# Attention and two mixtures of experts on one core: another place for the block means of v in SyncE's program

## The reference

```python
k_sum = k.reshape(B, H, nb, block, D).max(axis=3)
v_sum = v.reshape(B, H, nb, block, D).mean(axis=3)
scores_l = scale * np.matmul(q, k.transpose(0, 1, 3, 2))
mask_l = np.abs(pos[:, None] - pos[None, :]) < window
scores_s = scale * np.einsum('bhsd,bhnd->bhsn', q, k_sum)
scores_s = scores_s + np.log(block)
scores_l_m = np.where(mask_l, scores_l, -1000000000.0)
scores_all = np.concatenate([scores_l_m, scores_s], axis=-1)
scores_all = scores_all - np.max(scores_all, axis=-1, keepdims=True)
a = np.exp(scores_all)
a = a / (np.sum(a, axis=-1, keepdims=True) + 1e-09)
v_all = np.concatenate([v, v_sum], axis=2)
return np.matmul(a, v_all).astype(np.float32)
```

## Time and profile before

| what | us |
|---|---|
| median of 3 runs | 808.99 |
| lowest and highest | 808.78 and 811.25 |
| the profiled execution | 808.99 |
| its span, from the first to the last instruction | 806.9 |
| mean granted clock of TensorE | 0.945 |

### The profile page before, as it was taken

How to read it: one execution, slowest core, us unless ns; L and a number is a source line. 1 busy time by engine, 2 the same in 40 slices (tenths; PEclk the granted TensorE clock), 3 DMA queues, 4 the chain that set the end, 5 groups by cost and what they waited for, 6 DMA issues and landing times.

```text
span 806.9 us, 13908 instructions
## 1 busy us (share of the span) xinstructions
PE 727.3 (90%) x4566; PEld 504.6 (63%) x4566; DVE 361.3 (45%) x1477; ACT 219.8 (27%) x685; POOL 189.2 (23%) x253
## 2 busy tenths in 40 slices
PE   4789999998499999998239999999999999999995
PEld 3689999998387787675225455564555555455552
DVE  4477787977411111122774727456373654600000
ACT  3578787784011111111001021111111111021210
POOL 7465646632111111111010200202011020211001
PEclk7799999999599999999558999999999999999999
DMA  9799997686881528700051704307061250752001
GB/s 228 188 204 220 226 217 161 150 219 226 312 319 40 224 84 312 289 8 8 1 174 76 262 27 155 120 16 270 14 236 52 85 190 14 262 206 82 26 0 40
DMA packets 130483, 119.89 MB, mean 149 GB/s; under 512 B 95874, under 2 KB 95874, under 8 KB 130240
## 3 DMA queue, kind: packets, MB, share of 16 engines
q1 hardware_dynamic: 115312, 87.71, 35.6%
q10 hardware_dynamic: 9360, 15.47, 6.1%
q0 software_dynamic: 5760, 16.03, 5.7%
HBM read 105.95 MB, written 16.50 MB: 152 GB/s over the span
## 4 chain that ended last, share of the span: by engine, by line
PE 80%; DVE 8%; DMA 3%; issue 3%; SPq 2%; POOL 1%; ACTq 1%; ACT 0%; POOLq 0%; DVEq 0%
PE bank L1178 22%; PE bank L1193 21%; PE bank L1059 9%; PE bank L1076 9%; PE bank L912 4%; PE bank L933 3%; PE bank L1111 3%; PE bank L955 2%; PE bank L922 2%; DMA weights<-in_v 1%; DVE scratch L1409 1%; PE bank L1140 1%; DVE shared L1420 1%; PE bank L1039 1%; PE bank L899 1%
## 5 line engine op out<-in xcount | busy, mean ns | idle before, releaser
L1178 PE MATMUL bank<-scratch,weights 128*128 128x384 f32 x512 | 177.6, 499 | 0.1
L1193 PE MATMUL bank<-weights,scratch 128*128 128x512 f32 x384 | 175.2, 600 | 0.0
L1178 PEld LDWEIGHTS bank<-scratch,weights 128*128 128x128 f32 x512 | 94.5, 192 | 63.5 <-issue 10.1
L1193 PEld LDWEIGHTS bank<-weights,scratch 128*128 128x128 f32 x384 | 69.6, 190 | 70.7 <-issue 68.4
L1267 ACT ACTIVATE scratch<-shared,neg_max 128x120 f32<-128x120 f32 x192 | 73.4, 383 | 29.3 <-DVE neg_max L1420 18.1
L1371 ACT ACTIVATE scratch<-bank 128x384 f32<-128x384 f32 x64 | 31.4, 491 | 153.5 <-PE bank L1178 153.5
L689 POOL TENSOR_TENSOR scratch<-scratch,row_inv 128x480 f32<-128x480 f32 x48 | 47.3, 986 | 73.4 <-DVE row_inv L1430 73.1
L1059 PEld LDWEIGHTS bank<-mix,weights 128*128 128x128 f32 x512 | 60.5, 196 | 5.2 <-issue 5.2
L1059 PE MATMUL bank<-mix,weights 128*128 128x128 f32 x512 | 61.4, 279 | 1.4 <-DVE mix L1649 1.4
L850 POOL DMA_INDIRECT out<-scratch,idx x24 | 24.4, 1016 | 148.9 <-ACT scratch L1377 147.1
L1076 PE MATMUL bank<-weights,mix 128*128 128x512 f32 x128 | 58.2, 598 | 0.0
(11 more groups left out here) (245 smaller groups left out, 940.6 us busy)
## 6 DMA issues: line engine op xcount, KB each, us to landing
weights<-in_moe_w SPq DMA_DIRECT2D x20, 2048.0 KB, 7.7
scratch<-in_moe_w SPq DMA_DIRECT2D x8, 2048.0 KB, 10.8
weights<-in_moe_w ACTq DMA_DIRECT2D x16, 512.0 KB, 4.8
mix<-in_v SPq DMA_DIRECT2D x40, 192.0 KB
rows<-row SPq DMA_DIRECT2D x24, 264.5 KB, 3.6
scratch<-in_q SPq DMA_DIRECT2D x24, 256.0 KB, 4.6
weights<-in_k SPq DMA_DIRECT2D x21, 256.0 KB, 5.3
weights<-in_v ACTq DMA_DIRECT2D x24, 192.0 KB, 4.0
```

The lines of the kernel that those rows point to most:

```text
L1178: last = mm(hb2[f % 2][:, 0:CAP], w1_sb[odd][:, c, f * P:(f + 1) * P], xT2[odd][:, c, :], start=(c == 0), stop=(c == C - 1), skip_group_ch ...
L1193: last = mm(yb2[c % 2][:, :], hT2[odd][:, f, c * P:(c + 1) * P], w2_sb[odd][:, f, :], start=(f == 0), stop=(f == FC - 1), skip_group_check ...
```

## The change

The change reorders SP's loop over the tiles. `keep_means` now stands behind `store_tile` and `load_queries` of its step w = 4. The reads of the means into the next batch's buffers move from w = 4 to w = 5 and become four in one go, for n = 0 to 3, ahead of the k loads; only n = 4 and 5 keep theirs behind the window.

```diff
             for t in range(NT):
                 b, w = t // TB, t % TB
-                if w == 4 and b + 1 < B:
-                    keep_means(b + 1)
                 if t >= 2:
                     store_tile(t - 2)
                 if t + 4 < NT:
                     sp.wait_ge(s.q_turned, t + 2)
                     load_queries(t + 4)
+                if w == 4 and b + 1 < B:
+                    keep_means(b + 1)
+                if b + 1 < B and w == 5:
+                    sp.wait_ge(s.v_sum_out, 64 * (b + 2))
+                    for g in range(NH * (b + 1), NH * (b + 1) + 4):
+                        load_means(g)
                 if b + 2 < B:
                     for j in ((), (), (0,), (1,), (2, 3), (4, 5))[w] if b == 0 else (w,):
                         sp.wait_ge(s.k_turned, TB * b + j + 1)
                         load_k(b + 2, j)
-                if b + 1 < B and w == 4:
-                    sp.wait_ge(s.v_sum_out, 64 * (b + 2))
-                    for g in range(NH * (b + 1), NH * (b + 1) + 2):
-                        load_means(g)
                 for g in (2 * t + VR, 2 * t + 1 + VR):
                     if g < HT:
                         sp.wait_ge(s.attended, g - VR + 1)
                         load_window(g)
-                        if g >= NH and 2 <= g % NH < 6:
+                        if g >= NH and 4 <= g % NH < 6:
                             load_means(g)
```

## The result

| | before | after |
|---|---|---|
| median, us | 808.91 (8 runs) | 812.9 (8 runs) |
| lowest and highest | 807.66 and 811.25 | 812.0 and 815.98 |
| ratio, 95% interval | | 1.0052 (1.0035 to 1.0069) |
| profiled execution, span | 808.99, 806.9 | 818.46, 816.4 |

The change costs 4 us, 0.5%. The forecast was 809.1, and its range ended at 812.0: both were missed. The profiled execution lies above the runs of the table; 1.4 us of its difference to before arise ahead of the first moved line (DVE's copy of the earlier trace rows ended at 65.30 + 0.16, not 63.90 + 0.16), so I compare distances from there, not absolute times.

A forecast was written before the change was run, and what follows sets the result against it. PE was taken to bound the attention stage, waiting for nothing SyncE brings. All terms were 0 except 0.1 us for batch 1's first means: 808.99 + 0.1 = 809.1 us, range 807.9 to 812.0.

The forecast's parts named there:

- What bounds the kernel: Attention stage: PE busy 141.5 of 148.0 us, no wait for transfers after 47 us; reordering gains next to nothing.
- The early store and q: Step 4, batch 0: both issued 0.9 us earlier, gain 0; as a rival, 808.5 us at best, chance 0.05.
- Store, writes, and the moment of the reads: Batch 0: store at 64.1, writes from 65.1 to 68.4, reads of the next means issued at 71.9 to 73.9.
- Batch 3 free of loss: First product of batch 3: means issued at 157.65, wanted at 163.20, 5.5 us later; term 0.
- How long their 48 KB then take to land: First means of batch 1: landing between 73.8 and 79.4, need at 77.1, stall between 0 and 2.3 us.
- Where in this range? I count bytes: First means of batch 1: 1.89 MB at 253 GB/s, landing 75.9 to 77.8; stall 0 to 0.7, net 0.1 us.
- A middle value: First means of batch 1: landing at 76.9, middle of the byte count, just ahead of the need at 77.1.
- The upper bound: First means of batch 1: landing 5.5 us after issue, q's 5.0 plus half a microsecond, so 79.4 at the latest.
- the late means: Rival, chance 0.20: first means of batches 1 and 2 land late, stalls 2.3 and 0.6, net 2.1 us, so 811.1.
- The held issue: Rival, chance 0.09: first read's issue held by 2.4 us, stalls 4.2 and 2.5 in batches 1 and 2, 814.9 us.
- the refund that the prediction described: Behind batch 1's first product: up to 0.48 us of a stall paid back by PE's wait for DVE's copy of k.

The follow-up runs named there:

- reads later still: Against the changed kernel, the four reads of the means moved further back in step 5, behind the k loads too; 819.32 us, ratio 1.0132.

## Why the prediction was wrong

**What bounds the kernel: right.** PE bounds the stage, nothing that SP brought was waited for, and the change brought no gain. The early store and q were worth nothing, as argued; the kernel with only the writes late, in which they are just as early, stands at 0.9995.

**Store, writes, and the moment of the reads: right in batch 0.** The writes lasted 3.25 us against 3.24, and the reads began at 73.9 on the clock of before, in the reckoned 71.9 to 73.9. Batch 3 free of loss, k, q and later windows free of waits: right too. In batch 1 the reads began 8.9 us after the store of step 4 (122.77 - 113.85), not 7.2 (114.5 - 107.3): the writes took 0.4 us longer and the store of step 5, whose issue was held for 2.01 us, 1.7; the rest was a little shorter.

**The step that failed is "How long their 48 KB then take to land", with its answer "Where in this range? I count bytes".** It put the landing at 75.9 to 77.8 us. Measured, on the clock of before, it is 82.7 - 1.4 = 81.3 in one execution. What was wrong in it:

- The bytes themselves were nearly right. The counted 1.5 MB were through at 79.5 - 1.4 = 78.1, 0.3 us past the late edge: 2 us of near silence at the start, because the late writes let the queue run dry, and then all engines together at less than 253 GB/s.
- But the bytes say when the queue has moved so much in the sum, not when one transfer is complete. The twelve steps of the read's semaphore are spread over 2.7 us, from 79.98 to 82.70, while transfers issued behind it moved already; before, they were spread over 1.8 us (71.91 to 73.71). Why the last ones lag is not known.
- The issue was taken to be free. The first read was held for 2.01 us, against 0.55 before.
- A middle value was taken for a need that lay 0.2 us behind it, so any error on one side became a stall.

**The upper bound failed by the hold.** 5.5 us was q's landing of before plus a half; 7.4 were measured from the start of the read's issue, of which it spent 2.0 held; behind the hold 5.4 are left, just within the bound. The bound also borrowed its number from another queue: q itself took 5.0 in the earlier trace rows and 6.4 in the changed kernel.

Ten traces side by side, for the first read ahead of window 12 (us; "lands" is the last step of its semaphore):

| kernel | issue starts | issue lasts | lands | from start to landing | PE waits |
|---|---|---|---|---|---|
| before | 69.21 | 0.55 | 73.71 | 4.50 | 0 |
| changed | 75.27 | 2.01 | 82.70 | 7.43 | 4.11 |
| changed, again | 72.95 | 1.68 | 79.73 | 6.78 | 3.75 |
| k of step 5 behind the windows | 73.32 | 1.94 | 80.29 | 6.97 | 3.85 |
| change in batch 0 alone | 74.67 | 0.92 | 79.90 | 5.23 | 1.88 |
| only the reads late | 72.95 | 0.82 | 77.15 | 4.20 | 0.23 |
| reads ahead of the store | 72.15 | 0.50 | 76.56 | 4.41 | 0 |
| reads between store and q | 72.86 | 0.40 | 77.69 | 4.83 | 1.08 |
| k of step 4 behind the reads | 72.86 | 0.70 | 78.65 | 5.79 | 0.42 |
| reads later still | 81.13 | 2.21 | 85.58 | 4.45 | 4.47 |

In the second to the fifth row the same transfers stand ahead of the read in the same order, and it takes from 5.23 to 7.43 us: the longer the issue is held, the later it lands. Each row is one execution, and the start of an issue is itself put off by holds ahead of it, so the rows don't give a price per byte.

**The rule of the Trainium skill.** The Trainium skill, DMA: Bandwidth & Descriptors, Queues, rings and completion order, has each DMA engine consume a ring in order. The runs agree in direction: with the reads ahead of q or of both the medians lose little or nothing (809.53 and 808.47 us, against 812.9), and moving the k loads behind the reads still further back changed nothing (a wait of 3.85 us against 3.75). The byte count had already assumed this order, so the rule is not what was missing. What failed is the sentence that by it the sum is at most that of the late means, 811.1: that ceiling left out the hold and the clock.

**The rivals.** The held issue named the right places, nearly the right waits (4.2 and 2.5 us against 4.11 and 2.37) and the right mechanism: it had the first read out at 76.3 and landed at 81.3, and the trace has it out at 75.9 (77.28 - 1.4) and landed at 81.3. That its total, 814.9, missed the median of 812.9 is no wonder: the profiled execution is the slowest of its ten, and the others will have waited less, as the 1.88 us with the change in batch 0 alone suggest. I gave the case 0.09, on the argument that no hold shows behind windows, store and q; it does, as soon as they follow each other closely. The hold is not all of it: with q behind, where nothing was held (0.40 us), PE still waited 1.08 us. No run separates the hold from the queue, since the same full queue may be behind both.

**The clock was left out altogether.** After waits of 2.37 to 4.47 us PE went on at 0.50 of the clock for over 3 us, twice over 6, each costing about half its length by estimate: 1.6 to 3.3 us. In the profiled execution the two waits make 6.5 us, some 1.2 of them paid back by the waits for DVE's copies (2.3 us before, 1.1 after, the refund that the prediction described), and the two stretches of low clock add 3.2. That makes 8.5 us, against the 8.7 by which the stage's last product came later from the first moved line on (203.87 - 193.76 - 1.4). The median loss is only 4 us; smaller waits, and the clock in a part of the runs, would fit it, but only two executions of the changed kernel were traced.

## What to carry to other kernels

A small transfer that an engine waits for costs what stands ahead of it in its queue and how long its issue is held, not what it weighs. Put it ahead of the large ones: in this kernel the place of one 48 KB read per batch, ahead of 520 KB or behind them, was the whole difference between 812.9 and 809. A count of bytes gives the time when the sum of them is through, and here the last part of the read came 3 us later; nor does it hold the time that the issue is held. So where the reckoned landing lies within that distance of the need, forecast the stall, and price what the granted clock does behind it.

## What the runs showed of the hardware

Between 71.8 and 82.7 us of the changed kernel, with the engines full, SP's queue moved 2.03 MB, 186 GB/s, while all together moved 233; ACT's pieces had the rest, and most packets were under 512 bytes (6326 of 6798):

```profile
DMA packets 6798, 2.54 MB, mean 233 GB/s; under 512 B 6326, under 2 KB 6326, under 8 KB 6798
...
q1 hardware_dynamic: 6505, 2.03, 83.9%
```

One 48 KB read's issue took SP from 0.40 to 2.21 us, and its landing from 4.2 to 7.4 us from the start of the issue, by the table above. An idle PE of 2.37, 3.75, 4.11 and 4.47 us, in a stage otherwise full, was followed by stretches at 1.2 GHz of over 3 us; waits of 1.15, 1.88 and 1.91 us in other traces were not, as the stretches behind two of them show (the kernel with only the reads late, behind 1.91 us, and that with b = 0 alone, behind 1.88):

```profile
122.00:130.00 8.00, 7.88 (x71) 7.92 (x72) 4.30 (x27) 5.38 (x19) 2.24 (x3) 1.00 1.02 228
...
80.00:88.00 8.00, 8.00 (x72) 8.00 (x73) 4.42 (x27) 5.50 (x20) 2.27 (x3) 1.00 1.03 234
```

Executions of one and the same kernel differ in this by several microseconds, so that one trace with a short wait (1.15 us, 808.37) can stand for a kernel whose median is 812.09.
